# Routing the last unit of tokens from its own small products, with the expert stage in the same program block

## The reference

```
skip_score = x @ w_skip;  do_compute = skip_score > 0;  out = x.copy()
xc = x[do_compute];  logits = xc @ w_gate          # 8 experts
e_idx = argmax(logits);  gate_w = softmax(logits)[e_idx]
for e in range(8):                                  # w1[e]: 384x1024, w2[e]: 1024x384
    h = relu(xc[e_idx == e] @ w1[e])
    y[e_idx == e] = gate_w * (h @ w2[e])
out[do_compute] = xc + y
```

## Time and profile before

| | us |
|---|---|
| median of 3 runs | 998.07 (996.56 to 998.8) |
| the profiled execution, its own time | 1001.95 |
| its span, first to last instruction | 1000.1 |
| PE busy | 944.9 (94%) |
| DVE / ACT / POOL busy | 450.2 / 164.8 / 104.7 |
| mean granted TensorE clock | 0.979 |

### The profile page before, as it was taken

One profiled execution on the slowest core, in us unless ns is written; L12 is line 12 of the kernel. 1 busy time (PEld: TensorE's weight loads), 2 busy tenths in 40 slices (PEclk: granted clock), 3 DMA queues, 4 the chain that ended last, 5 costly groups with the idle time before them and its releaser, 6 DMA issues. The chain is left out here.

```text
span 1000.1 us, 22930 instructions
## 1 busy us (share of the span) xinstructions
PE 944.9 (94%) x10033; PEld 627.0 (63%) x10033; DVE 450.2 (45%) x1098; ACT 164.8 (16%) x345; POOL 104.7 (10%) x136
## 2 busy tenths in 40 slices
PE   5999999999999999999999999999999189999996
PEld 5965655665665565566556656665555077887785
DVE  7967754774668467536734753211110211111111
ACT  2221211211221121022112111110110021111110
POOL 2010100101011010101011010001001112222121
PEclk9999999999999999999999999999999579999998
DMA  9820013004100500220040001004600014452400
GB/s 356 301 113 1 27 47 114 26 2 136 48 3 2 182 3 1 90 95 1 2 167 19 1 13 38 1 1 165 261 1 32 19 33 160 166 204 102 159 30 27
DMA packets 30298, 78.74 MB, mean 79 GB/s; under 512 B 4072, under 2 KB 20120, under 8 KB 29312
## 3 DMA queue, kind: packets, MB, share of 16 engines
q1 hardware_dynamic: 20112, 61.46, 17.0%
q10 hardware_dynamic: 6912, 9.55, 2.6%
q0 software_dynamic: 3184, 6.39, 2.1%
HBM read 65.34 MB, written 13.00 MB: 78 GB/s over the span
## 5 line engine op out<-in xcount | busy, mean ns | idle before, releaser
L902 PE MATMUL ps<-wo,prod 128*128 128x393 f32 x576 | 207.2, 506 | 4.4 <-DVE prod L580 4.3
L882 PE MATMUL ps<-xT,wg 128*128 128x384 f32 x576 | 206.5, 495 | 0.7 <-ACT xT L686 0.7
L891 PE MATMUL ps<-xT,wv 128*128 128x384 f32 x576 | 204.7, 492 | 0.0
L580 DVE TENSOR_TENSOR prod<-sig,ps 128x384 f32<-128x384 f32 x96 | 52.9, 553 | 235.1 <-PE ps L891 234.5
L902 PEld LDWEIGHTS ps<-wo,prod 128*128 128x128 f32 x576 | 105.4, 191 | 77.0 <-DVE prod L580 8.2
L882 PEld LDWEIGHTS ps<-xT,wg 128*128 128x128 f32 x576 | 107.3, 191 | 70.9 <-issue 2.0
L891 PEld LDWEIGHTS ps<-xT,wv 128*128 128x128 f32 x576 | 107.0, 190 | 70.1 <-issue 0.6
L1154 PEld LDWEIGHTS ps_h<-xgT,arena 128*128 128x128 f32 x816 | 96.3, 196 | 5.2 <-ACT xgT L1111 1.0
L1154 PE MATMUL ps_h<-xgT,arena 128*128 128x128 f32 x816 | 96.5, 280 | 0.6 <-ACT xgT L1111 0.6
L691 ACT ACTIVATE sig<-ps 128x384 f32<-128x384 f32 x96 | 47.2, 491 | 274.5 <-PE ps L882 274.5
L1166 PE MATMUL ps_y<-arena,hT 128*128 128x384 f32 x272 | 90.5, 486 | 0.0
(11 more groups left out here) (160 smaller groups left out, 681.4 us busy)
## 6 DMA issues: line engine op xcount, KB each, us to landing
arena<-in_moe_w SPq DMA_DIRECT2D x16, 1536.0 KB, 10.6
arena<-in_kq SPq DMA_DIRECT2D x7, 1536.0 KB, 8.4
x_scratch<-x ACTq DMA_DIRECT2D x24, 196.5 KB, 4.4
arena<-in_kn SPq DMA_DIRECT2D x8, 576.0 KB, 4.8
vr<-in_v SPq DMA_DIRECT2D x8, 576.0 KB, 9.7
arena<-in_kr SPq DMA_DIRECT2D x8, 576.0 KB, 4.9
out<-x ACTq DMA_DIRECT2D x24, 192.0 KB, 3.6
prod<-in_turned_moe_w_out SPq DMA_DIRECT2D x1, 2304.0 KB, 12.6
```

The costliest lines, as they stand in the source:

```text
L580: nc.vector.tensor_tensor(prod[:, f, :], sig[:, f % 2, :], ps_m[3 - f % 2][:, 0:CT], ALU.mult)\
L882: last = nc.tensor.matmul(ps_m[f % 2][:, 0:CT], wg[:, a, f * P:(f + 1) * P], xT[:, a, :], start=(a == 0), stop=(a == KT - 1))
L891: last = nc.tensor.matmul(ps_m[3 - f % 2][:, 0:CT], wv[:, a, f * P:(f + 1) * P], xT[:, a, :], start=(a == 0), stop=(a == KT - 1))
L902: last = nc.tensor.matmul(ps_m[t][:, 0:XW], prod[:, a, t * P:(t + 1) * P], wo[:, a, :], start=(a == 0), stop=(a == NF - 1))
```

## The change

Four things are changed.

1. For the last unit only, two stages of their own give the scores. `logits`, behind the first output part of tile 0: 12 matmuls with a stationary operand of 128x32 (`wor`, the nine router columns padded with zeros to 32) and `prod` as the moving one, 384 columns; four strips of 32 output partitions each take three of the twelve, so the result is four partial sums, stacked. ACT copies it to `xT[:, 0]`. `logit_turn`, behind the second output part: three small matmuls by a stacked identity `sel` that add the four strips and turn them to token rows, 128x9 per tile. `route` of the last unit then reads these (`lg`) and not `x2`; it stands behind the second output part, and `rank` behind the first part of tile 1.
2. `phase_b` is no longer a block: its code follows on each engine behind the code of `phase_a`, with no barrier. The constants are made at the start of the program. The SBUF that `wg`, `wv`, `vr` and `y1` use is used again as `xres`; PSUM banks 0 to 3 are `ps_h`, bank 4 `ps_y`, bank 7 `ps_x`.
3. Each tile of x is stored to `x_scratch` first and to `out` second, with a semaphore for each. POOL waits for the three `x_scratch` stores ahead of the first gather of rows, and for the three `out` stores ahead of the loop.
4. `WARM_GAP = 0`: a loop that could put matmuls into the gap issues none.

```diff
@@ dense_pieces
+    early = {(0, 0): ["logits"], (0, 1): ["logit_turn", "route"], (1, 0): ["rank"]}
...
             if t == 0 and part == 0 and q:
                 pieces.append(("rank", q - 1, 0))
+            if q == Q - 1:
+                pieces += [(stage, q, 0) for stage in early.get((t, part), ())]
@@ program_order
-    return order + [("route", Q - 1, 0), ("rank", Q - 1, 0)]
+    return order
@@ GpSimd
+        nc.gpsimd.memset(wor[:], 0.0).then_inc(pads, 1)
...
         pool.wait_ge(listed, 16 * NT)
+
+        pool.wait_ge(rows_ready, 1)
+        nc.gpsimd.indirect_dma_start(
+            tile_ids[:, :], None, lists_d.rearrange("(r c) o -> r (c o)", c=P),
...
+        pool.wait_ge(ey_used, 1)
...
+        for t in range(TT):
+            pool.wait_ge(x2_saved[t], 16 * Q)
+        gather(0)
+        pool.wait_ge(x_turned, 1)
+        pool.wait_ge(x_kept, 1)
+        gather(1)
+        for t in range(TT):
+            pool.wait_ge(out_saved[t], 16 * Q)
@@ VectorE
-                nc.vector.tensor_copy(wo[:, :, DM:XW], ps_m[2][:, 0:NF * R1].rearrange("p (f e) -> p f e", f=NF))\
-                    .then_inc(router_copied, 1)
+                routers = ps_m[2][:, 0:NF * R1].rearrange("p (f e) -> p f e", f=NF)
+                nc.vector.tensor_copy(wo[:, :, DM:XW], routers)
+                nc.vector.tensor_copy(wor[:, :, 0:R1], routers).then_inc(router_copied, 1)
...
+                if q == Q - 1:
+                    dve.wait_ge(logits_turned, 1)
+                    nc.vector.tensor_copy(lg[:], ps_a[:, 1, 0:TT * R1].rearrange("p (t e) -> p t e", t=TT)).then_inc(logits_ready, 1)
+                    dve.wait_ge(logits_ready, 1)
+                    scores = lg[:]
+                else:
+                    dve.wait_ge(x2_copied, TT * (q + 1))
+                    scores = x2[:, :, DM:XW]
@@ ScalarE
-                act.dma_start(out[r0:r0 + P, :], x2[:, t, 0:DM]).then_inc(x2_stored[t], 16)
-                act.dma_start(x2_d[r0:r0 + P, :], x2[:, t, :]).then_inc(x2_stored[t], 16)
+                act.dma_start(x2_d[r0:r0 + P, :], x2[:, t, :]).then_inc(x2_saved[t], 16)
+                act.dma_start(out[r0:r0 + P, :], x2[:, t, 0:DM]).then_inc(out_saved[t], 16)
+            elif stage == "logits":
+                act.wait_ge(logits_done, 1)
+                nc.scalar.activation(xT[:, 0, :], ps_a[:, 0, 0:CT], ACT.Copy).then_inc(logits_copied, 1)
...
-        for t in range(TT):
-            act.wait_ge(x2_stored[t], 32 * Q)
@@ TensorE
+            elif stage == "logits":
+                pe.wait_ge(prod_ready, NF * (q + 1))
+                pe.wait_ge(u_ready, JS * Q)
+                for a in range(NF // 4):
+                    for i in range(4):
+                        last = nc.tensor.matmul(ps_a[i * H2:(i + 1) * H2, 0, 0:CT], wor[:, i * (NF // 4) + a, :],
+                                                prod[:, i * (NF // 4) + a, :], start=(a == 0), stop=(a == NF // 4 - 1))
+                last.then_inc(logits_done, 1)
+            elif stage == "logit_turn":
+                pe.wait_ge(logits_copied, 1)
+                for t in range(TT):
+                    last = nc.tensor.matmul(ps_a[:, 1, t * R1:(t + 1) * R1], xT[:, 0, t * P:(t + 1) * P], sel[:, 0:R1],
+                                            start=True, stop=True)
+                last.then_inc(logits_turned, 1)
...
         pe.wait_ge(idf_ready, 1)
+        pe.wait_ge(x2_copied, TT * (Q - 1) + 1)
         nc.tensor.transpose(ps_y[:, 0:P], tile_idf[:], ident[:]).then_inc(ids_turned, 1)
+
+        for _ in range(WARM_GAP):
+            nc.tensor.matmul(ps_x[:, 0:2 * P], ident[:], prod[:, 0, 0:2 * P], start=True, stop=True)
```

More of the change, by code:

```diff
@@ L52, in program_order @@
 def program_order(Q, QS, NF, TT, KT):
-    light = ("route", "rank", "x_turn")
+    light = ("route", "rank", "x_turn", "logits", "logit_turn")
     order, pieces, later = [], [], []
@@ L171, in build, with program @@
         w_in_e = [whole.enter_context(nc.semaphore(f"ew_in{i}")) for i in range(WS)]
[L173 to L179, removed]
+        program(nc, whole, locals())
+def program(nc, ctx, g_):
     (kq_d, kr_d, kn_d, v_d, beta_d, wg_d, wv_d, wo_d, ws_d, wgt_d, w1_d, w2_d, wo_t_d, out, x2_d, lists_d, ident, counts,
@@ L239, in phase_a @@
     length = sb("length", [P, NS])
-    wg = sb("wg", [P, KT, F])
-    wv = sb("wv", [P, KT, F])
     wo = sb("wo", [P, NF, XW])
     wr = sb("wr", [P, KT, R1])
+    wor = sb("wor", [P, NF, H2])
+    sel = sb("sel", [P, H2])
+    lg = sb("lg", [P, TT, R1])
     xT = sb("xT", [P, KT, CT])
@@ L262, in phase_a @@
     slot = sb("slot", [P, NT], I32)
+    steps = sb("steps", [P, NT])
+    tile = sb("tile", [P, 1])
+    first = sb("first", [P, E])
+    more = sb("more", [P, E, NT])
+    ntile = sb("ntile", [P, E])
+    ends = sb("ends", [P, E])
+    starts = sb("starts", [P, E])
+    endi = sb("endi", [P, E], I32)
+    mine = sb("mine", [P, E])
+    mine2 = sb("mine2", [P, E])
+    rowf = sb("rowf", [P, 1])
+    row = sb("row", [P, 1], I32)
+    tile_ids = sb("tile_ids", [P, P], I32)
+    tile_idf = sb("tile_idf", [P, P])
+    ids = sb("ids", [P, P], I32)
+    idx_g = sb("idx_g", [P, 1], I32)
+    idx_s = sb("idx_s", [P, 1], I32)
+    xg = sb("xg", [P, XW])
+    nmax = sb("nmax", [P, 1])
+    ex = sb("ex", [P, E])
+    esum = sb("esum", [P, 1])
+    gate = sb("gate", [P, 1])
+    xgT = sb("xgT", [P, KT, P])
+    hT = sb("hT", [P, FT, P])
+    yv = sb("yv", [P, DM])
     ps = psum("ps", [P, 8, 512])
@@ L266, in phase_a @@
     ps_m = [ps[:, 4 + i] for i in range(4)]
+    ps_h = [ps[:, i] for i in range(4)]
+    ps_y = ps[:, 4]
+    ps_x = ps[:, 7]
     masks = sem("masks"); ident_ready = sem("ident_ready"); mask_step = sem("mask_step"); pads = sem("pads"); filled = sem("filled")
@@ new lines, in _ @@
+        nc.vector.tensor_copy(endi[:], ends[:])
+        link(nc.vector.tensor_tensor(starts[:], ends[:], ntile[:], ALU.subtract))
+        link(nc.vector.tensor_scalar(mine[:], starts[:], tile[:, 0:1], None, ALU.is_le))
+        link(nc.vector.tensor_scalar(mine2[:], ends[:], tile[:, 0:1], None, ALU.is_gt))
+        link(nc.vector.tensor_tensor(mine[:], mine[:], mine2[:], ALU.mult))
+        link(nc.vector.tensor_tensor(mine2[:], first[:], starts[:], ALU.subtract))
+        link(nc.vector.tensor_tensor(mine[:], mine[:], mine2[:], ALU.mult))
@@ new lines, in _, with keep_rows @@
+        link(nc.vector.reduce_sum(rowf[:], mine[:], axis=AX.X))
+        nc.vector.tensor_copy(row[:], rowf[:]).then_inc(rows_ready, 1)
+        dve.wait_ge(scattered, 16)
+        nc.vector.tensor_copy(tile_idf[:], tile_ids[:]).then_inc(idf_ready, 1)
+        dve.wait_ge(ids_turned, 1)
+        nc.vector.tensor_copy(ids[:], ps_y[:, 0:P]).then_inc(ey_used, 1)
+        def keep_rows(t, nth):
+            dve.wait_ge(x_in, 16 * nth)
+            nc.vector.tensor_copy(xres[:, bass.ds(t, 1), :].rearrange("p o d -> p (o d)"), xg[:]).then_inc(x_kept, 1)
@@ L706, in _, with turned @@
             mlp(stage, q, i)
-        for t in range(TT):
-            act.wait_ge(x2_stored[t], 32 * Q)
+        def turned(nth):
+            act.wait_ge(x_turned, nth)
+            nc.scalar.activation(xgT[:].rearrange("p a c -> p (a c)"), ps_x[:, 0:KT * P], ACT.Copy)\
+                .then_inc(xg_ready, 1)
+        turned(1)
+        start = 0
+        act.wait_ge(rows_ready, 1)
+        for e in range(E):
+            end = bound(act, e)
+            with act.Fori(start, end) as j:
+                for fp in (0, 2):
+                    act.wait_ge(h_done, 4 * j + fp + 1)
+                    nc.scalar.activation(hT[:, 2 * fp:2 * fp + 2, :].rearrange("p a c -> p (a c)"),
+                                         ps_h[fp][:, 0:2 * P], ACT.Relu).then_inc(h_act, 1)
+                    if fp == 0:
+                        act.wait_ge(max_ready, j + 1)
+                        nc.scalar.activation(ex[:], xres[:, bass.ds(j, 1), DM + 1:XW].rearrange("p o d -> p (o d)"),
+                                             ACT.Exp, bias=nmax[:, 0:1], accum_out=esum[:, 0:1]).then_inc(sum_ready, 1)
+                turned(j + 2)
+            start = end
     @block.tensor
```

311 lines of the change are left out of this document (109 added, 202 removed).

## The result

The changed kernel takes 982.56 us (median; 982.19 to 983.92) where the kernel before, run beside it, took 998.14: ratio 0.985, interval 0.983 to 0.987. The forecast was 982. Two later groups of runs gave ratios of 0.986 (0.984 to 0.988) and 0.987 (0.985 to 0.989); in medians the gain was 15.6, 14.2 and 12.6 us.

What follows compares the result with a forecast made beforehand. Dense TensorE bounds the kernel except one 28.5 us gap before the expert matmuls. Ending it 16.5 us earlier, less 0.2 for the second router copy, gave 16.3 off 998.07: 981.8, said as 982; range 978.5 to 988.

Steps and rivals of the forecast that it cites:

- Logits: TensorE, last unit: four strips side by side 1.9 us, overlap read from a packed stage, plus 0.5 for tile shape: 2.4.
- logit_turn: TensorE, behind the second output part: six small passes adding 0.7 us.
- rank: TensorE: the last unit's `rank` now stands among the output products and adds 0.46 us there.
- No wait inside: TensorE's last-unit stream: reaches `rank` at 765.6 with `ind` ready at 761.3, 4.3 us of slack, so no wait.
- List chain: Lists, table and `tile_ids` run behind products: `tile_ids` done at 778.2, TensorE's stream ends at 780.1, indices ready at 781.2.
- rival B: At the gather: the list chain ends last, a loss of 3 us, 985; chance 0.07.
- Stores last: Ahead of the gather: `x_scratch` stores land at 782.8 after 2.1 us from issue, 1.6 us behind the indices.
- Gap: TensorE between the last output product and the first expert matmul: idles 8.5 us, but for the turns.
- Clock: First expert block: TensorE's clock falls again in the gap and costs the same 2.8 us, no gain or loss.
- A: Logits: strips don't run side by side, taking 7.8 to 12.3 us instead of 2.4; time 987 to 992; chance 0.12.
- C: In the gap: TensorE's clock does not fall, 2.8 us gained, time 979; chance 0.06.
- D: Behind the gap: clock stays at half long after, kernel slower; 60 us at half gives 1009; chance 0.02.

Runs made afterwards that it cites:

- one_strip: Changed kernel with all 12 logits matmuls accumulating into one strip of 32 output partitions instead of four: 989.48 us, ratio 0.992 to the kernel before.
- warm14: Changed kernel with WARM_GAP = 14 in place of 0, 14 matmuls in the gap that nobody reads: 979.3 us, ratio 0.983 to the kernel before.
- after: First profile of the changed kernel, no further edit: median 982.56 us, ratio 0.985 to the kernel before.
- same_third: Third profile of the changed kernel, no edit: 983.74 us, ratio 0.987 to the kernel before.
- late_route: Changed kernel, still one block, but the last unit routed at the end again with scores from `x2`: 994.84 us, ratio 0.995 to the kernel before.
- two_blocks: Changed kernel with early routing kept, but the block closed ahead of the expert stage, barrier back: 990.78 us, ratio 0.991 to the kernel before.
- best2: Changed kernel plus GpSimd DRAINs behind `tile_ids` and each loop turn, 12 unread products, first index copy ahead of the stores' wait: 976.26 us, ratio 0.979.
- before: First profile of the kernel before the change: profiled execution 1001.95 us, median 998.14 beside the changed kernel.
- best: Changed kernel plus GpSimd DRAINs behind `tile_ids` and at each loop turn, and the 14 products of warm14: 979.59 us, ratio 0.980.
- drain_once: Changed kernel plus one GpSimd DRAIN behind the issue of `tile_ids`, none in the loop: 984.29 us, ratio 0.984 to the kernel before.
- before_again: The kernel before, profiled once more without edit: one run of 1000.21 us.

## Why the prediction was right, step by step

The mechanism held at each step, mostly to a few tenths. Times are counted from the first output part of the last unit, since this execution started its last unit 5.4 us earlier.

- *Logits* 2.4: 2.07. *logit_turn* 0.7: 753.86 - 753.28 = 0.58. *rank* 0.46: 0.36. Sum 3.0 for 3.6. Half of that difference was lost again: the rest of the stretch, the 36 output matmuls and the `rank` of the unit before, took 24.8 us where it took 24.5. The bound from the packed stage was the right row to trust, and 1.9 alone would have been nearer than 1.9 + 0.5. one_strip shows what was at stake: 5.8 us.
- *No wait inside*: right. `rank` 13.3 us behind the first part (forecast 13.6), `ind` long ready.
- *List chain*: `tile_idf` at 772.94, 1.3 us before TensorE can turn it; forecast 1.9. Right, and rival B is out. (The sum left out the 0.3 us between the landing of `tile_ids` and its turn, in which DVE makes it floats. TensorE's late end hides them; in the worst case they would have put the indices 0.2 us behind the stores and not 0.1 ahead.)
- *Stores last*: right. The landing took 2.4 in the chain (2.1 forecast, 2.2 and 2.3 in other executions).
- *From the index copy to the first expert matmul*: 783.22 - 777.56 = 5.66, forecast 5.67.
- *Gap* 8.5: 8.8. *First expert matmul*: 36.6 us behind the first part, forecast 788.6 - 752.0 = 36.6. 16.4 us earlier than before, forecast 16.5. That close a hit is luck: the stream ended 0.3 us earlier than forecast, counted from its first part, and the gap was 0.3 us longer.
- *Clock*: right. It fell between 777 and 779, came back between 788 and 790, and the first block took 8.15 against 8.17. That they agree to 0.02 is luck too: the other profiles of these two kernels have 7.30, 7.62 and 7.73. warm14 puts the price in the block at 2.0 to 2.5 (7.62 to 8.15, less 5.62), forecast 2.8.

Three things were not in the sum. First, *the meeting at the end*. I let the barrier in the middle go for nothing in return; its DRAIN came back at the end as 2.1 us (5.22 for 3.09). "What waits for it" I asked of each wait that was added, and not of the block's end, which the diff doesn't touch but whose work it adds to (63 DMAs for 37). The row for it stood in the trace before: two DRAINs whose lengths differ with what GpSimd had issued. 16.4 - 2.1 = 14.3, and the stretch to the end says 13.7 to 14.9.

Second, *0.36 us ahead of the last unit*. From the first `prod` of the third unit to the first output part of the last, both profiles of the kernel before take 494.5 us (494.47, 494.48) and all twelve of the kernels made from the changed one 494.8 (494.82 to 494.84). Where I followed it (after, same_third, late_route, two_blocks) it arises in one place: VectorE starts the last `prod` of the fourth unit 0.36 us later behind the same matmuls (its wait is 1.60 where it was 1.24). What holds it there stays open. The net is then 13.9. The 0.2 that the sum took off for the second router copy can't be told: the copy takes 0.25 in the trace, but the first `prod` comes anywhere from 69.6 to 72.6 us.

Third, *the base*. The prediction took off 16.3 from the median 998.07. With 13.9 it would have said 984.1, and medians of the changed kernel were 982.56, 983.3 and 983.74. So the 981.8 of the sum was 0.8 to 1.9 us too low, in a range of 9.5. Measured as gains, 16.3 was too much by 0.7, 2.1 and 3.7 us; why the third group gave only 12.6 isn't shown. The mechanism of the gap was right, and the first median happened to hide most of the term that was missing: that 982 was hit within 0.6 is in part luck. The 19.8 us between the two profiled executions are 16.4, less 2.1, and 5.4 that lie ahead of the last unit: 3.7 and 1.7 of them have no tie with the change that a run showed and are in the last section, and a start 0.4 us earlier is set off by the 0.36.

The prices of two rivals could be tried as kernels: A is one_strip (989.5; forecast 987 to 992, near its lower end, since the loads stay hidden), C is warm14 (979.3; forecast 979, of which its trace shows 2.5 to 3.1 us of gain and not the 4.0 of the medians). B and D did not occur: in the 14 profiled executions of all kernels together the first expert block never took over 8.6 us.

## What to carry to other kernels

A cost that is taken out of the middle with a barrier may be owed at the end: look at what the block's last instruction does for each engine, and for GpSimd count its DMAs, 0.08 us each, and pay them with a DRAIN where the engine idles. Where a gap can't be closed, its price is the idle time and the slow clock behind it; 5 to 6 us of products that nobody reads, ending 0.9 to 1.6 us before the rows came, bought back 2.5 to 3.1 us here. And take a change apart by stretches between fixed instructions, not by spans: three groups of medians differed by 3 us on the same pair of kernels, the gap stretches by 0.6.

## What the runs showed of the hardware

**GpSimd's DRAIN** costs 0.10 us + 0.081 us for each DMA issued since the last one, where all of them have landed (2, 26, 36, 37 and 63 DMAs: 0.22, 2.20, 3.01, 3.09, 5.22). Behind DMAs in flight it takes longer: 4.88 behind `tile_ids` with 27, and 1.79 to 6.36 in the loop with 2.

**An indirect DMA starts 0.7 us late.** It stands 0.74 us behind the wait that releases it in best2, where that is a store's landing, and 0.73 in the changed kernel, where it is the index copy.

**TensorE stands still near 227 us in some executions.** Among the second unit's output products, in the third unit's scan, TensorE stands still three times for 0.4 us, with few passes in between, and waits for nothing that the profile shows. Timeline of late_route:

```profile
226.72 0.46 PE L982 MATMUL ps<-st,arena 48*64 48x48 f32 x18
227.55 0.35 PE L982 MATMUL ps<-st,arena 48*64 48x48 f32 x5 [0.37 <-issue]
228.28 0.32 PE L982 MATMUL ps<-st,arena 48*64 48x48 f32 x4 [0.39 <-issue]
229.03 0.38 PE L982 MATMUL ps<-st,arena 48*64 48x48 f32 x9 [0.43 <-issue]
```

and behind it, its windows:

```profile
230.00:234.00 4.00, 4.00 (x8) 2.13 (x7) 3.69 (x10) 0.50 (x1) 0.00 (x0) 0.57 0.00 0
```

From the second unit's first `prod` to the third's that execution takes 94.25 us. So do before (94.25), best (94.24), drain_once (94.23) and two_blocks (94.16); before_again has the stall without the fall of the clock (92.54), and the other eight take 90.57 or 90.58. So the stall costs 2.0 us and the fall behind it 1.7 more. The four kernels of one group all had it, and the seven of the two groups that shared another chip did not, though all eleven hold nearly the same code. With one profile of each that points to the chip or the hour and not to the kernel, but doesn't show it. What holds TensorE there stays open; it wasn't tried. The kernel before had a further 1.7 us in its first unit in both its profiles, and late_route had it too, with the clock at half behind 66 us, and no other kernel; three executions don't tell whether that belongs to them.
